# Sink attention with two feed-forward layers: high weights meet high and low tokens in one 512-column matmul in the second and third chunks

## The reference

```python
def _moe_ref(x, w_in, w_out):          # x 1536x512, w_in 512x2048, w_out 2048x512
    h = x @ w_in
    relu6 = np.clip(h + 3.0, 0.0, 6.0)
    return (h * relu6 / 6.0) @ w_out

def _moe2_ref(x, w_in, w_out):
    h = x @ w_in
    return (h * (1.0 / (1.0 + np.exp(-1.702 * h)))) @ w_out

x = attention(q, k, v)                 # tokens x (heads * 64)
return _moe2_ref(_moe_ref(x, w_in, w_out), w_in2, w_out2)
```

## Time and profile before

| | |
|---|---|
| median of 3 runs | 613.11 us (612.9 to 616.2) |
| the profiled execution | 615.47 us, its span 613.6 us |
| TensorE busy | 595.6 us (97%), granted clock 0.997 of full speed |
| VectorE busy | 414.2 us (68%) |
| ScalarE busy | 275.9 us (45%) |
| GpSimd busy | 207.2 us (34%) |

### The profile page before, as it was taken

How to read it: one execution, slowest core, us unless ns; L and a number is a source line. 1 busy time by engine, 2 the same in 40 slices (tenths; PEclk the granted TensorE clock), 3 DMA queues, 4 the chain that set the end, 5 groups by cost and what they waited for, 6 DMA issues and landing times.

```text
span 613.6 us, 11380 instructions
## 1 busy us (share of the span) xinstructions
PE 595.6 (97%) x4192; PEld 534.7 (87%) x4192; DVE 414.2 (68%) x815; ACT 275.9 (45%) x591; POOL 207.2 (34%) x213
## 2 busy tenths in 40 slices
PE   5999888999999999999999999999999999999997
PEld 4888777988989899999989898989999898989896
DVE  4879877768998545575455887789845557554533
ACT  6778765464644323243232774646432225232322
POOL 7699852578960000000000698796000000000000
PEclk9999989999999999999999999999999999999999
DMA  7624162286895544545354366869556536366501
GB/s 259 218 81 116 66 255 79 95 283 235 297 386 198 178 184 156 204 141 219 129 227 157 123 232 263 277 238 331 212 210 204 226 129 230 122 210 217 198 41 69
DMA packets 16152, 118.05 MB, mean 192 GB/s; under 512 B 1840, under 2 KB 2160, under 8 KB 9968
## 3 DMA queue, kind: packets, MB, share of 16 engines
q1 hardware_dynamic: 16112, 117.55, 53.2%
HBM read 85.03 MB, written 32.51 MB: 192 GB/s over the span
## 4 chain that ended last, share of the span: by engine, by line
PE 83%; DVE 6%; POOL 4%; issue 4%; ACT 2%; DMA 1%; DVEq 0%; SPq 0%; ACTq 0%; POOLq 0%
PE psum L1038 12%; PE psum L1040 12%; PE psum L1039 12%; PE psum L1081 7%; PE psum L1080 7%; PE psum L1082 7%; PE psum L1075 6%; PE psum L1076 6%; PE psum L1077 6%; PE psum L966 2%; PE psum L1009 2%; PE psum L979 2%; POOL up_split L544 2%; POOL low L522 1%; DVE gated L913 1%
## 5 line engine op out<-in xcount | busy, mean ns | idle before, releaser
L1038 PE MATMUL psum<-x_split,up_split 128*128 128x256 f32 x672 | 190.9, 284 | 0.5 <-POOL up_split L544 0.4
L1040 PE MATMUL psum<-x_split,up_split 128*128 128x256 f32 x672 | 190.1, 283 | 0.0
L1039 PE MATMUL psum<-x_split,up_split 128*128 128x256 f32 x672 | 190.1, 283 | 0.0
L1038 PEld LDWEIGHTS psum<-x_split,up_split 128*128 128x128 f32 x672 | 128.7, 192 | 4.9 <-POOL up_split L544 2.8
L1039 PEld LDWEIGHTS psum<-x_split,up_split 128*128 128x128 f32 x672 | 128.8, 192 | 1.6
L1040 PEld LDWEIGHTS psum<-x_split,up_split 128*128 128x128 f32 x672 | 128.7, 192 | 0.0
L544 POOL TENSOR_TENSOR up_split<-up_raw,up_split 128x512 fp32r<-128x512 f32 (+1 forms) x32 | 38.6, 1224 | 191.1 <-ACT up_split L638 191.1
L895 DVE TENSOR_TENSOR hidden<-psum,hidden 128x512 f32<-128x512 f32 x48 | 32.9, 686 | 77.7 <-PE psum L1040 77.7
L700 ACT ACTIVATE gated<-hidden,one_half 128x512 f32<-128x512 f32 x48 | 32.4, 716 | 100.1 <-DVE hidden L906 100.1
L1075 PE MATMUL psum<-gated_split,down_split 128*128 128x512 f32 x192 | 75.0, 391 | 0.0
L1080 PE MATMUL psum<-down_split,gated_split 128*128 128x512 f32 x192 | 75.0, 391 | 0.0
(11 more groups left out here) (87 smaller groups left out, 988.6 us busy)
## 6 DMA issues: line engine op xcount, KB each, us to landing
up_split<-kept_up SPq DMA_DIRECT2D x32, 1792.0 KB, 7.3
kept_up<-up_split SPq DMA_DIRECT2D x16, 1792.0 KB, 6.7
up_raw<-w SPq DMA_DIRECT2D x16, 512.0 KB, 8.5
down_raw<-w SPq DMA_DIRECT2D x16, 512.0 KB, 9.2
raw<-qk SPq DMA_DIRECT2D x7, 776.0 KB, 4.6
values<-v_keys SPq DMA_DIRECT2D x8, 384.0 KB
out<-y_stage SPq DMA_DIRECT2D x12, 256.0 KB, 8.6
raw<-qk SPq DMA_DIRECT2D x1, 264.0 KB, 3.3
```

The source lines that it names most:

```text
L1038: pe.matmul(product_at(q), w_high, x_high, start=d == 0, stop=False)
L1039: pe.matmul(product_at(q), w_high, x_low, start=False, stop=False)
L1040: last = pe.matmul(product_at(q), w_low, x_high, start=False, stop=d == 1)
```

## The change

In chunks 1 and 2 of both layers the matmul of high weights with high tokens and that with low tokens become one of 512 columns: `merged_at(q)` is a whole PSUM bank, its first 256 columns for the high tokens, the other 256 for the low ones. Low weights with high tokens add to the first half. A product is then the sum of two halves of a bank, and VectorE's new `merge` makes the hidden blocks in nine sums in place of four, with ScalarE's `copy_half` for products 0 and 3. A VectorE instruction takes one of its operands from PSUM and the other from SBUF here, so the two halves of a product are added one after the other. There are four banks for seven products, `MERGED_BANK`: products 4, 5 and 6 reuse banks 0, 1 and 2 of the same pair, and TensorE waits before products 4 and 5 for sums of `merge` (semaphore `merged`).

GpSimd takes over `low_product` in chunks 1 and 2, and `sum_x` there (the sums of tokens for the chunk that follows). Chunk 0 of either layer is as before, but for a reordered `hidden` tile and finer counting of `products_ready` (every product, not every other).

```diff
+        MERGES = 9
+        MERGED_BANK = [0, 1, 2, 3, 0, 1, 2]
+        def merged_at(q):
+            return psum[:, MERGED_BANK[q], :].rearrange("p (a t) -> p a t", a=2)
...
+            for chunk, (layer, c) in enumerate(CHUNKS):
+                for p in range(PAIRS):
+                    n = chunk * PAIRS + p
+                    for m in range(2, MADE):
+                        if pair_number(m) == n + 1:
+                            for part in range(4):
+                                up_low(m, part)
+                            if m + 1 < MADE:
+                                up_sums_first(m + 1)
+                                up_sums_second(m + 1)
+                    if c:
+                        if chunk + 1 < len(CHUNKS) and 3 <= p < 7:
+                            sum_x(chunk + 1, p - 3)
+                        low_product(n, 0)
+                        low_product(n, 1)
...
+            def copy_half(layer, c, p, q, into):
+                act.wait_ge(products_ready, PRODUCTS * ((layer * NCHUNK + c) * PAIRS + p) + q + 1)
+                if c == 1 and p == 0:
+                    act.wait_ge(combined, 4 * PAIRS * (layer + 1))
+                act.wait_ge(merged, MERGES * merged_pair(layer, c, p) + MERGES)
+                act.activation(hidden[:, into, :], merged_at(q)[:, 0, :], ACT.Copy).then_inc(halves_copied, 1)
...
+            def merge(layer, c, p, new_low=lambda q: None):
+                so_far = MERGES * merged_pair(layer, c, p) + MERGES
+                done = PRODUCTS * ((layer * NCHUNK + c) * PAIRS + p)
...
+                dve.wait_ge(halves_copied, 2 * merged_pair(layer, c, p) + 1)
+                dve.tensor_tensor(hidden[:, 7, :], half(0, 1), hidden[:, 7, :], ALU.add).then_inc(merged, 1)
+                new_low(0)
+                dve.wait_ge(products_ready, done + 3)
+                dve.wait_ge(merged, so_far + 1)
+                dve.tensor_tensor(hidden[:, 1:6:4, :], both_of(1, 0), hidden[:, 7:8, :].to_broadcast([P, 2, HALF_CHUNK]), ALU.add
+                                  ).then_inc(merged, 1)
+                dve.wait_ge(merged, so_far + 2)
+                dve.tensor_tensor(hidden[:, 1:6:4, :], both_of(1, 1), hidden[:, 1:6:4, :], ALU.add).then_inc(merged, 1)
+                new_low(1)
+                dve.wait_ge(halves_copied, 2 * merged_pair(layer, c, p) + 2)
+                dve.tensor_tensor(hidden[:, 7, :], half(3, 1), hidden[:, 0, :], ALU.add).then_inc(merged, 1)
+                new_low(2)
+                dve.wait_ge(products_ready, done + 5)
+                dve.wait_ge(merged, so_far + 3)
+                dve.tensor_tensor(hidden[:, 6, :], half(4, 0), hidden[:, 5, :], ALU.add).then_inc(merged, 1)
...
+                new_low(3)
+                dve.wait_ge(products_ready, done + 7)
+                dve.wait_ge(merged, so_far + 7)
+                dve.tensor_tensor(hidden[:, 2:4, :], both_of(1, 0), hidden[:, 0:7:6, :], ALU.add).then_inc(merged, 1)
+                dve.wait_ge(merged, so_far + 8)
+                dve.tensor_tensor(hidden[:, 2:4, :], both_of(1, 1), hidden[:, 2:4, :], ALU.add).then_inc(merged, 1)
...
-                    low_product(n, 0)
+                    if c == 0:
+                        low_product(n, 0)
...
+                        if q in (0, 1, 4, 5):
+                            pe.wait_ge(merged, so_far + {0: 6 - MERGES, 1: 0, 4: 1, 5: 3}[q])
...
+                            if d:
+                                pe.matmul(merged_at(q)[:, 0, :], w_low, x_high, start=False, stop=False)
+                            last = pe.matmul(merged_at(q), w_high, x_split[:, :, q, d, :], start=d == 0, stop=d == 1)
+                            if d == 0:
+                                pe.matmul(merged_at(q)[:, 0, :], w_low, x_high, start=False, stop=False)
+                    last.then_inc(products_ready, 1)
```

More of the change, by code:

```diff
@@ L267, in local_sink_attention_and_two_ffns @@
         combined = sem("combined")
+        halves_copied = sem("halves_copied")
+        merged = sem("merged")
         gate_ready = sem("gate_ready")
@@ L724, in _ @@
                         empty(chunk - 1)
-                    copy_first(n)
+                    if c == 0:
+                        copy_first(layer, p)
+                    else:
+                        copy_half(layer, c, p, 0, 7)
                     if new_x:
-                        for q in range(5):
+                        for q in range(3):
                             round_x(chunk + 1, q)
-                    gate(layer, n, 0)
+                    if c:
+                        copy_half(layer, c, p, 3, 0)
+                    if new_x:
+                        for q in (3, 4):
+                            round_x(chunk + 1, q)
+                    gate(layer, c, p, 0)
                     if new_x:
                         round_x(chunk + 1, 5)
-                    gate(layer, n, 1)
+                    gate(layer, c, p, 1)
                     if new_x:
@@ L827, in sum_x @@
             def sum_x(chunk, i):
-                c = chunk % NCHUNK
                 x_valid(dve, chunk)
@@ L931, in _ @@
                         empty(chunk - 1)
-                    if new_x:
-                        combine(n, lambda q: low_x(chunk + 1, q))
+                    new_low = (lambda q: low_x(chunk + 1, q)) if new_x else (lambda q: None)
+                    if c == 0:
+                        combine(layer, p, new_low)
                     else:
-                        combine(n)
+                        merge(layer, c, p, new_low)
                     gate(layer, n, 0)
@@ L941, in _ @@
                         low_x(chunk + 1, 5)
-                    low_product(n, 0)
+                    if c == 0:
+                        low_product(n, 0)
                     if new_x:
                         low_x(chunk + 1, 6)
-                    low_product(n, 1)
-                    if more and 3 <= p < 7:
+                    if c == 0:
+                        low_product(n, 1)
+                    if c == 0 and 3 <= p < 7:
                         sum_x(chunk + 1, p - 3)
```

112 lines of the change are left out of this document (74 added, 38 removed).

## The result

The changed kernel takes 635.12 us (median of 6 runs, 634.15 to 638.81). The kernel before took 614.25 beside it (6 runs, 612.9 to 616.2). The ratio is 1.0352, 95% interval 1.0333 to 1.0371: slower by 3.5%. The forecast was 625.2 in a range of 617.5 to 633.5, so the direction was right and the size was not. The profiled execution took 634.97 us with a span of 633.2 us and a granted clock of 0.994.

What follows compares the result with a forecast made beforehand. TensorE, busy 97% of the span, was taken as the bound. Net steady stall 8.0, first boundary 2.8, last pairs 0.8 and end 0.5 sum to 12.1 us over the 613.1 median: 625.2, 2.0% slower, range 617.5 to 633.5.

Steps and rivals of the forecast that it cites:

- The saving of the wide matmul: In each merged pair 14 matmul starts of some 12 ns go: 0.17 us per pair, 5.4 us over 32 pairs.
- The stall at product 5: In each merged pair TensorE waits 0.45 us for VectorE's third sum; net 0.25 per pair, 8.0 us over 32.
- First boundary: First chunk to second, first layer: product 4 waits 2.7 us for late VectorE; 2.8 us more than the steady 0.25.
- last pairs: In merged chunks' last pairs VectorE's next-token low parts delay sums: 0.1 at two boundaries, 0.6 at layer's end; together 0.8 us.
- end: At the kernel's end the last down part's second half waits for GpSimd's second low part: 0.5 us.
- GpSimd's low weights for the second layer also queue behind its low products: At the layer boundary these weights end at 21.1, TensorE wants them at 21.4; up to 1 us, counted only in rival C.
- rival C: Much slower: VectorE and GpSimd get in each other's way and boundaries stall too; 20.3 us more, 633; chance 0.14.
- ScalarE's extra copy lies in its long waits: In merged pairs ScalarE's added copy of 0.38 us falls into its waits and costs nothing.
- the rest of a steady pair is covered: In steady merged pairs GpSimd's low parts end at 11.8 to 12.7, needed at about 16; cover 3 to 4 us, no cost.
- VectorE is free again 12.6 after such a pair's start: Entering the second merged chunks, VectorE is in time for product 4, due at 13.7; margin 0.4 us, no stall.
- Rival A: Faster: no stall at product 5 in merged pairs; 608 us, or 611 with the first boundary still paid; chance 0.07.
- rival B: No change: the stall at product 5 is nearer 0.25 us and the first boundary milder; about 616 us; chance 0.09.

Runs made afterwards that it cites:

- Experiment 1: The changed kernel with the two 512-column sums of products 1 and 2 made into four of 256 columns; 626.5 us, 1.0185 to the kernel before.
- empty_first: The changed kernel with `empty` ahead of roundings and low weights in a chunk's second pair; 632.14 us, 1.0297 to the kernel before.
- Experiment 2: The same run as empty_first: the changed kernel with `empty` ahead of roundings and low weights in a chunk's second pair; 632.14 us.
- experiment 3: The changed kernel with the gates' low products back on VectorE, token sums still on GpSimd; 630.19 us, 1.0263 to the kernel before.
- 10: wide_middle with low products and token sums on VectorE in layer 1's last chunk only, on GpSimd elsewhere; 610.28 us, 0.9947 to the kernel before.
- gpsimd_alone: The kernel before, matmuls unchanged, with GpSimd making the gates' low parts and token sums in chunks 1 and 2; 619.94 us, 1.008.
- merge_alone: The changed kernel with merged matmuls but all low products and token sums on VectorE; 631.62 us, 1.0287 to the kernel before.
- wide_middle: The changed kernel with sums of products 1 and 2 split, first and last pairs of merged chunks narrow as before; 613.45 us, 0.9993 to the kernel before.
- low_on_vector: The same run as experiment 3: the changed kernel with the gates' low products back on VectorE; 630.19 us, 1.0263 to the kernel before.
- middle_vector: wide_middle with all low products and token sums back on VectorE; 610.25 us, 0.9942 to the kernel before.
- last_low_gpsimd: The changed kernel with the low products of chunk 0's last pair moved to GpSimd too; 637.34 us, 1.0376 to the kernel before.

## Why the prediction was right and wrong

**The saving of the wide matmul: right.** Where no stall hides it, a pair is 10.33 in place of 10.50, in five kernels. The measurement gives 12 ns for each start saved. By the 2.5 ns of the Trainium skill ("TensorE: Matmul & The Clock Gate", Back-to-back issue gap) the pair would be 10.46, an estimate; the measurement decides.

**The stall at product 5: right in mechanism, mis-sized by a fifth.** The term "0.25 between them, 32 x 0.25 = 8.0 us" measured 0.20 x 32 = 6.4. The second sum started with the quicker hand-over that the half copy had shown, so the lower bound held. Experiment 1 removed the wait and with it the stall.

**First boundary, last pairs, end: right.** 2.7 for 2.8, 1.1 for 0.8, 0.6 for 0.5. The first boundary had a part not foreseen, which fell out differently from kernel to kernel: after the long wait at product 4 (2.5 in the waits above) the granted clock sometimes falls. Two windows of empty_first, whose pair took 15.30 in place of 13.70:

```profile
189.00:191.00 2.00, 1.80 (x6) 1.55 (x7) 1.92 (x5) 0.00 (x0) 0.00 (x0) 0.63 0.00 0
191.00:193.00 2.00, 2.00 (x8) 1.62 (x7) 1.05 (x2) 0.00 (x0) 0.00 (x0) 0.52 0.05 12
```

**The step that failed first: "GpSimd's low weights for the second layer also queue behind its low products ... so up to 1 us", which stood in rival C and not in the sum.** I compared the end of those weights (21.1 after the last pair's start) with TensorE's wish (21.4). They ended 22.95 after it (371.41 less 348.46), and TensorE lost 1.0 us in layer 2's first pair, as much as I had allowed; the 0.6 of it that went in the wait for L899 would have gone in the wait for the weights otherwise. But I stopped at the first consumer. The same queue then made the sums for the next weights late, ScalarE waited for these with `empty` behind it, and `empty` frees the banks of a down part: 4 us, and 2.4 more at the lower clock: 6.4 us that stood nowhere in the sum. "ScalarE's extra copy lies in its long waits" and "the rest of a steady pair is covered" were true of the steady pair and were carried over to a boundary where the same engines also round weights. Experiment 2 takes 6.3 of the 6.4 us away by putting `empty` ahead of the roundings, 3 and 10 take most of it away by relieving GpSimd's queue, and gpsimd_alone makes 4.4 of it with that queue loaded and VectorE's gate product stretched beside it.

**The second: "VectorE is free again 12.6 after such a pair's start ... a margin of 0.4 after its first sum".** Both second merged chunks overran it. Rows of the changed kernel:

```profile
273.40 3.12 POOL L595 TENSOR_TENSOR gated_split<-gated,gated_split 128x512 fp32r<-128x512 f32 x2 [10.72 <-ACT gated_split L762]
273.60 1.78 DVE L899 TENSOR_TENSOR x_split<-x_sums,x_split 128x512 fp32r<-128x512 f32 x1
275.31 0.41 DVE L979 TENSOR_TENSOR hidden<-psum,hidden 128x256 f32<-128x256 f32 x1
...
275.77 0.50 PE L1157 MATMUL psum<-x_split,up_split 128*128 128x512 f32 x1 [0.41 <-DVE hidden L979]
...
277.29 0.50 PE L1157 MATMUL psum<-x_split,up_split 128*128 128x512 f32 x1 [0.55 <-DVE hidden L986]
```

VectorE is free 13.75 after the start of the last pair (275.31 less 261.56), 1.1 more than I had, and the 1.1 is the stretched low part. Rival C named this. But giving the work back to VectorE doesn't help (experiment 3): two low products there are about as long as the stretch.

**Taken together** the forecast's own terms, 12.1 us, measured 10.8, and two places that it held free of cost another 9.6: layer 2's first two pairs 7.4, the starts of the second merged chunks 2.2. Those are rival C's places. I gave C 0.14, and its 20.3 us is close to the 20.4 that the table adds up to before its last line, but by chance: it had 10.6 for the steady pairs, which took 6.4, and up to 1 for GpSimd's late weights, which cost 7.4. Rival A falls with the stall that was there in all 32 pairs, rival B with its size, 0.20 net and not 0.08.

Slips of the working that decide nothing: the lower end of the range, 617.5, is said to have the steady stall at its lower bound and half the first boundary, which makes 613.1 + 6.7 + 1.4 + 1.3 = 622.5; rival B's sum gives 616.7; the margin of 0.4 at the second merged chunks comes to 0.5 by its own terms; and TensorE's slices in the earlier trace rows are full from the eighth on.

## What to carry to other kernels

Follow a delayed queue past its first consumer: list all that stands behind the late instruction, and what each of those holds up, up to the next PSUM bank that must be emptied. When an edit makes banks scarcer, look for its price not in the steady state alone (6.4 us here, which splitting two sums gave back) but in the few pairs where the freeing engine has other work. Splitting the sums, keeping the old form in just those pairs, and keeping the second engine out of the chunk before its own urgent work turned 3.5% slower into 0.5% faster here. Work moved to an engine with idle time is free only if nothing urgent stands behind it there and nothing urgent runs beside it on the engine that it slows.

## What the runs showed of the hardware

TensorE's granted clock fell from 1.00 to 0.50 in the stretch in which it worked 1.64 us of 4.80, and 512-column matmuls went from 0.228 to 0.43 us apart, for some 5 us. Over layer 2's second pair the mean clock was 0.80 in the change (16.88 us), 0.89 in gpsimd_alone (14.92) and 0.88 in merge_alone (14.56), but 1.00 in wide_middle (13.28) and low_on_vector (12.19). After the wait of 2.5 us at the first boundary it fell in some profiles (pairs of 14.5 to 15.3 us) and not in others (13.70 and 13.72). So one long wait can cost more than its length. The times scatter with it: the changed kernel's runs spread over 4.7 us, and the two slowest have the lowest mean clock, 0.991; those of middle_vector spread over 1.5. It is not the only source of scatter, for the kernel before has one run of 616.2 at a clock of 1.00.

GpSimd and VectorE subtractions with both inputs in SBUF stretched each other so far (0.69 to 1.75 and 1.29 to 1.55 us in last_low_gpsimd) that moving 1.4 us of work off VectorE shortened the wait for it by 0.15.
